# The expert stage in groups of 400 rows instead of 384, with the dense stage left at 384

## What is computed

```python
# x: 3072 tokens x 384, from the attention
logits = x @ w_gate + modality_bias[modality_id]      # 8 experts, 2 modalities
e_idx = np.argmax(logits, axis=1)
for e in range(8):                                    # w1[e]: 384 x 1024, w2[e]: 1024 x 384
    mask = e_idx == e
    h = np.maximum(x[mask] @ w1[e], 0.0)
    out[mask] = gate_w[mask, None] * (h @ w2[e])
# dense stage on all tokens, d_ff = 1536
g = x @ w_gate;  val = x @ w_val
y = (silu(g) * val) @ w_out
```

## Time and profile before

| | us |
|---|---|
| median of three runs | 1021.41 |
| lowest and highest | 1020.64, 1023.75 |
| the profiled execution, its time on the device | 1021.33 |
| its span, first to last instruction | 1019.6 |
| mean granted TensorE clock | 0.975 |

### The profile page before, as it was taken

The page is one execution under the profiler, slowest core; times in us unless marked ns, Lnnn a source line. Parts: engine busy times, 40 slices in busy tenths (PEclk is TensorE's granted clock), DMA queues, the critical chain, the costliest instruction groups (busy, mean ns, idle before and its releaser), DMA issues.

```text
span 1019.6 us, 15885 instructions
## 1 busy us (share of the span) xinstructions
PE 936.1 (92%) x6100; PEld 888.9 (87%) x6100; DVE 579.2 (57%) x993; ACT 382.2 (37%) x536; POOL 175.6 (17%) x198
## 2 busy tenths in 40 slices
PE   2688999999959999999999999999999999999994
PEld 0566878888839999999998999999999999999994
DVE  6978777755566666666555445544444444535432
ACT  7987878756434545444342110111101111011110
POOL 6234234531842211100000001010101000010101
PEclk9799999999959999999999999999999999999998
DMA  9998743420368987765454000000101000000000
GB/s 170 156 156 117 112 88 49 63 56 1 126 215 273 331 280 249 248 201 173 153 187 136 1 24 24 24 24 3 45 1 47 1 24 24 24 24 1 24 1 23
DMA packets 211487, 98.83 MB, mean 97 GB/s; under 512 B 150854, under 2 KB 206406, under 8 KB 211403
## 3 DMA queue, kind: packets, MB, share of 16 engines
q1 hardware_dynamic: 197994, 70.19, 30.3%
q0 software_dynamic: 4368, 14.75, 4.2%
q10 hardware_dynamic: 9040, 12.78, 3.9%
HBM read 77.58 MB, written 20.08 MB: 96 GB/s over the span
## 4 chain that ended last, share of the span: by engine, by line
PE 79%; ACT 5%; DVE 5%; issue 5%; DMA 2%; SPq 2%; POOL 1%; ACTq 0%; DVEq 0%; POOLq 0%
PE psum L1759 27%; PE psum L1771 15%; PE psum L1714 9%; PE psum L1727 9%; PE psum L1568 4%; PE psum L1577 3%; PE psum L1558 2%; PE psum L1613 2%; PE psum L1547 2%; PE psum L1594 2%; PE psum L1616 1%; SPq L587 1%; PE psum L1549 1%; PE psum L1701 1%; ACT group_work L1482 1%
## 5 line engine op out<-in xcount | busy, mean ns | idle before, releaser
L1759 PE MATMUL psum<-xT_parts,w_parts 128*128 128x384 f32 x1728 | 316.3, 335 | 2.3 <-DVE xT_parts L1210 2.3
L1759 PEld LDWEIGHTS psum<-xT_parts,w_parts 128*128 128x128 f32 x1728 | 302.3, 189 | 2.6 <-issue 2.6
L1218 DVE TENSOR_TENSOR group_work<-group_work,psum 128x384 f32<-128x384 f32 x96 | 53.2, 554 | 233.1 <-ACT group_work L1526 233.1
L1526 ACT ACTIVATE group_work<-psum 128x384 f32<-128x384 f32 x96 | 47.2, 492 | 355.3 <-PE psum L1759 355.3
L1771 PE MATMUL psum<-w_parts,act_parts 128*128 128x384 f32 x864 | 166.3, 335 | 5.7 <-DVE act_parts L1226 5.7
L1771 PEld LDWEIGHTS psum<-w_parts,act_parts 128*128 128x128 f32 x864 | 150.7, 188 | 8.4 <-DVE act_parts L1226 8.4
L1714 PE MATMUL psum<-xT_parts,expert_parts 128*128 128x384 f32 x648 | 129.3, 344 | 5.4 <-DVE expert_parts L1167 4.5
L1727 PE MATMUL psum<-act_parts,expert_parts 128*128 128x384 f32 x648 | 123.9, 335 | 0.4 <-DVE act_parts L1172 0.4
L1714 PEld LDWEIGHTS psum<-xT_parts,expert_parts 128*128 128x128 f32 x648 | 113.4, 191 | 8.4 <-DVE expert_parts L1167 6.7
L1727 PEld LDWEIGHTS psum<-act_parts,expert_parts 128*128 128x128 f32 x648 | 112.9, 188 | 1.1 <-DVE act_parts L1172 0.8
L569 POOL DMA_INDIRECT out<-group_work,sorted_id x24 | 23.6, 981 | 462.3 <-ACT group_work L1532 457.4
(11 more groups left out here) (192 smaller groups left out, 1041.6 us busy)
## 6 DMA issues: line engine op xcount, KB each, us to landing
group_work<-in_w SPq DMA_DIRECT2D x160, 192.0 KB, 3.5
group_work<-xs_scratch SPq DMA_DIRECT2D x10, 576.0 KB, 4.7
yT_scratch<-group_work ACTq DMA_DIRECT2D x9, 576.0 KB, 4.4
arena<-in_q SPq DMA_DIRECT2D x24, 192.0 KB, 4.0
arena<-in_k SPq DMA_DIRECT2D x24, 192.0 KB, 4.2
arena<-in_v SPq DMA_DIRECT2D x24, 192.0 KB, 4.4
x_scratch<-x_all SPq DMA_DIRECT2D x24, 192.0 KB, 1.9
xs_scratch<-group_work POOLq DMA_DIRECT2D x8, 576.0 KB, 5.9
```

Of the source, the lines that this page charges most:

```text
L1218: link(nc.vector.tensor_tensor(sig[:, w % 2, :], sig[:, w % 2, :], psum[:, w % 2, 0:GW], ALU.mult))
L1759: last = nc.tensor.matmul(psum[:, b, 0:GW], wt[:, i, k, f * P:(f + 1) * P], x_p[:, j, g % 2, k, :], start=(k == n == 0), stop=(k == KC - 1 ...
```

## The change

- The expert stage has groups of `GE` = `GW` + 16 = 400 rows: matmuls with 400 columns, and ScalarE's and VectorE's operations on `psum`, `x_p` and `act_p` with them. `x_p`, `act_p`, the padding of the scratch tensors and the result buffer `y_sb` (its memory still shared with `osb`) grow; the table is worked out with 400.
- The rows of a group are three tiles of 128 and one of 16 (`xg_last`, sharing memory with `sig`). GpSimd gathers a fourth tile for group 0 and stores it too; the later rounds gather tiles 4 to 6, 7 to 9 and so on, the last one two tiles. `load_rows` has a second DMA of 16 rows. TensorE does a fourth transpose of 16 rows in each `xtr`.
- GpSimd has seven more small operations behind the table, which count the groups that begin in the first 384 columns (times 16), into `tab[3]`.
- The load of the dense stage's first group moves from GpSimd to SyncE, behind all weight loads and behind the nested `If`s of groups 9 and up. It waits for all rows to be sorted and for as many stores as `tab[3]` says.
- The dense stage keeps its 384 columns.

```diff
+    EXTRA = 16
+    GE = GW + EXTRA
...
-                link(nc.gpsimd.tensor_single_scalar(group_pos[:], group_iota_f[:], float(GW), ALU.mult))
+                link(nc.gpsimd.tensor_single_scalar(group_pos[:], group_iota_f[:], float(GE), ALU.mult))
...
-            nc.gpsimd.tensor_copy(tab[0:1, 2, 0:1], sums[:, 1, NE - 1:NE]).then_inc(s_tab, 1)
+            nc.gpsimd.tensor_copy(tab[0:1, 2, 0:1], sums[:, 1, NE - 1:NE])
+            link(nc.gpsimd.memset(begin[:], 0.0))
+            link(nc.gpsimd.tensor_scalar(begin[:, 0:MG], group_at[:], float(GW), 16.0, ALU.is_lt, ALU.mult))
+            half = 8
+            while half >= 1:
+                link(nc.gpsimd.tensor_tensor(begin[:, 0:half], begin[:, 0:half], begin[:, half:2 * half], ALU.add))
+                half //= 2
+            nc.gpsimd.tensor_copy(tab[0:1, 3, 0:1], begin[:, 0:1]).then_inc(s_tab, 1)
...
-            for i in range(TG):
-                pool.indirect_dma_start(xg[:, 0, i], None, x_dram[:, :],
+            for i in range(TG + 1):
+                pool.indirect_dma_start(x_tile(0, i), None, x_dram[:, :],
...
-            pool.wait_ge(s_yst, 16 * NE)
-            pool.dma_start(yT_in, yT_dram[:, 0:GW].rearrange("(k p) n -> p k n", p=P)).then_inc(s_gl0, 16)
+            pool.sem_inc(s_sorted, 1)
...
+                sp.dma_start(xg_last[0:EXTRA, t % 2], xs_dram[ds(first + GW, EXTRA), :]).then_inc(s_xl[t % 2], 16)
...
+            needed = sp.value_load(tab[0:1, 3, 0:1], min_val=16, max_val=16 * NE)
+            sp.wait_ge(s_sorted, 1)
+            sp.wait_ge(s_yst, needed)
+            sp.dma_start(yT_in, yT_dram[:, 0:GW].rearrange("(k p) n -> p k n", p=P)).then_inc(s_gl0, 16)
             stored(NG - 1)
             more_groups(sp, total, NG, NG, stored)
...
-                nc.scalar.activation(act_p[:, 0, w % 2], psum[:, w % 2, 0:GW], ACT.Relu).then_inc(s_hs, 1)
+                nc.scalar.activation(act_p[:, 0, w % 2], psum[:, w % 2, 0:GE], ACT.Relu).then_inc(s_hs, 1)
...
+            def transpose_rows(t, k, i):
+                rows = P if i < TG else EXTRA
+                return nc.tensor.transpose(psum[:, x_bank(t, k), i * P:i * P + rows],
+                                           x_tile(t % 2, i)[0:rows, k * P:(k + 1) * P], ident[0:rows, 0:rows])
...
-                        last = nc.tensor.matmul(psum[:, w % 2, 0:GW], we_p[:, w % SLOTS, i, k * P:(k + 1) * P],
+                        last = nc.tensor.matmul(psum[:, w % 2, 0:GE], we_p[:, w % SLOTS, i, k * P:(k + 1) * P],
                                                 x_p[:, j, t % 2, k, :], start=(k == n == 0),
```

More of the change, by code:

```diff
@@ L81, in build @@
         sorted_id = sb("sorted_id", [P, NT], U32)
-        tab = sb("tab", [1, 4, 32], I32)
+        tab = sb("tab", [1, 4, 16], I32)
         phase = ExitStack()
@@ L302, in build @@
         s_zero = sem("xs_zeroed")
-        s_xf = [sem(f"first_rows{i}_gathered") for i in range(TG)]
+        s_xf = [sem(f"first_rows{i}_gathered") for i in range(TG + 1)]
         s_xs0 = sem("first_rows_stored")
         s_srt = sem("x_rows_sorted")
+        s_sorted = sem("all_rows_sorted")
         s_xs = sem("sorted_rows_stored")
@@ L363, in x_turn, with sorted_tiles, x_tile @@
             return (t + 1, at.index(f)) if f in at and t + 1 < MG else None
+        def sorted_tiles(t):
+            return min(NT, (t + 1) * TG + 1)
+        def x_tile(slot, i):
+            return xg[:, slot, i] if i < TG else xg_last[:, slot]
         w1_v = w1.rearrange("e (k p) f -> p e k f", p=P)
@@ L528, in _ @@
             nc.gpsimd.tensor_copy(tab[0:1, 0, 0:MG], group_e[:]).then_inc(s_te, 1)
-            link(nc.gpsimd.tensor_scalar(small[:, 1, :], sums[:, 0], float(-GW), None, ALU.mult))
+            link(nc.gpsimd.tensor_scalar(small[:, 1, :], sums[:, 0], float(-GE), None, ALU.mult))
             link(nc.gpsimd.tensor_tensor(small[:, 1, :], small[:, 1, :], small[:, 0, :], ALU.add))
@@ L1131, in _ @@
             link(nc.vector.tensor_tensor(small[:, 0, :], cum[0:1, 1:NE + 1], cum[0:1, 0:NE], ALU.subtract))
-            link(nc.vector.tensor_scalar(sums[:, 0], small[:, 0, :], 1.0 / GW, (GW - 1) / 2 / GW, ALU.mult, ALU.add))
+            link(nc.vector.tensor_scalar(sums[:, 0], small[:, 0, :], 1.0 / GE, (GE - 1) / 2 / GE, ALU.mult, ALU.add))
             link(nc.vector.tensor_scalar(sums[:, 0], sums[:, 0], ROUND, -ROUND, ALU.add, ALU.add))
@@ L1207, in split @@
                         dve.wait_ge(s_gv, FFC * (g - 1))
-                high, low = x_p[:, 0, g % 2, k], x_p[:, 1, g % 2, k]
+                high, low = x_p[:, 0, g % 2, k, 0:GW], x_p[:, 1, g % 2, k, 0:GW]
                 link(nc.vector.tensor_copy(high, yT_in[:, k]))
@@ L1223, in _ @@
                         dve.wait_ge(s_o, w - 1)
-                    high, low = act_p[:, 0, w % 2], act_p[:, 1, w % 2]
+                    high, low = act_p[:, 0, w % 2, 0:GW], act_p[:, 1, w % 2, 0:GW]
                     link(nc.vector.tensor_copy(high, sig[:, w % 2]))
@@ L1487, in y_out @@
                     act_e.wait_ge(s_yst, 16 * t)
-                act_e.dma_start(yT_dram[:, ds(first, GW)].rearrange("(k p) n -> p k n", p=P), osb[:, t % 2]
+                act_e.dma_start(yT_dram[:, ds(first, GE)].rearrange("(k p) n -> p k n", p=P), y_sb[:, t % 2]
                                 ).then_inc(s_yst, 16)
@@ L1686, in _ @@
             last.then_inc(s_ids, 1)
+            def transpose_rows(t, k, i):
+                rows = P if i < TG else EXTRA
+                return nc.tensor.transpose(psum[:, x_bank(t, k), i * P:i * P + rows],
+                                           x_tile(t % 2, i)[0:rows, k * P:(k + 1) * P], ident[0:rows, 0:rows])
             def first_rows():
-                for i in range(TG):
+                for i in range(TG + 1):
                     pe.wait_ge(s_xf[i], 16)
                     for k in range(KC):
-                        last = nc.tensor.transpose(psum[:, x_bank(0, k), i * P:(i + 1) * P],
-                                                   xg[:, 0, i, k * P:(k + 1) * P], ident[:])
-                        if i == TG - 1:
+                        last = transpose_rows(0, k, i)
+                        if i == TG:
                             last.then_inc(s_xTp, 1)
             def xtr(t, k):
-                pe.wait_ge(s_xl[t % 2], 16 * ((t + 1) // 2))
+                pe.wait_ge(s_xl[t % 2], 32 * ((t + 1) // 2))
                 pe.wait_ge(s_xT, t * KC + k)
-                for i in range(TG):
-                    last = nc.tensor.transpose(psum[:, x_bank(t, k), i * P:(i + 1) * P], xg[:, t % 2, i, k * P:(k + 1) * P], ident[:])
+                for i in range(TG + 1):
+                    last = transpose_rows(t, k, i)
                 last.then_inc(s_xTp, 1)
@@ L1726, in down @@
                     for n, (i, j) in enumerate(PRODUCTS):
-                        last = nc.tensor.matmul(psum[:, 4 + k, 0:GW], we_p[:, w % SLOTS, i, at:at + P],
+                        last = nc.tensor.matmul(psum[:, 4 + k, 0:GE], we_p[:, w % SLOTS, i, at:at + P],
                                                 act_p[:, j, w % 2], start=(f == n == 0),
```

47 lines of the change are left out of this document (26 added, 21 removed).

## The result

The changed kernel takes 1028.41 us, the median of 20 runs (1024.73 to 1034.04), beside 1021.85 us (1020.64 to 1027.18, 20 runs) for the kernel before: 1.0064 times as long, 95% interval 1.0047 to 1.0080. The forecast was 1014.9 us. The profiled execution took 1027.27 us, with a span of 1025.5. So the change, which takes away a group of 26.7 us, costs 6.6 us.

The account below looks back on a forecast made before the run. TensorE, 92% busy, was taken to bound the kernel; -26.7 + 7.7 + 2.6 + 1.25 + 0.2 - 0.5 + 8.4 + 0.6 = -6.45 us from 1021.33 gave 1014.9 us, range 1009 to 1019.5.

Parts of the forecast that it names:

- What bounds the kernel: TensorE, busy for 92% of the span; dense stage untouched by the change, so the whole question is when it starts.
- Part 1, the ninth group: Expert stage: 400 rows a group need eight groups instead of nine, so the ninth goes; -26.7 us.
- Part 2, sixteen columns: Expert stage: each of 1152 matmuls takes 6.67 ns more for sixteen more columns; +7.7 us (bounds 0 and 8.3).
- 400 columns are a bad width: Rival, at each of the 1152 expert matmuls: paced as if 448 columns, 26.7 ns more, 1038 us; chance 0.06.
- Part 3, the fourth transpose: Expert stage: 24 more transposes on TensorE at 0.11 us each; +2.6 us (bounds 0 and 2.6).
- Part 4, the start: Group 0's fourth gather delays the first `up` by 1.25 us; group 1's rows come later, +0.2 us.
- Part 5, inside each group: Waits of `up` at group ends: cover grows by 0.12 us, the chain by 0.05; -0.5 us over seven.
- Part 6, the handover: Before the dense stage: yT_in's load behind SyncE's weight loads and jump, idle 10.8 us against 2.32; +8.4 us.
- Part 7, the clock: First dense matmuls: lower granted clock after the long handover gap; +0.6 us (bounds -1.0 and +2).

Follow-up runs that it names:

- b_rows400: The kernel before with only the rows of x_p and act_p 400 elements (1600 bytes) apart, still nine groups of 384 columns; 1028.6 us, 1.0068 of before.
- a_align: The changed kernel with rows of x_p 1792 and act_p 2048 bytes apart, single output buffer to make room; 1022.7 us, 0.9989 of before.
- a_16first: The changed kernel with the 16-row transpose issued ahead of the three full ones instead of behind them; 1026.9 us, 1.0054 of before.
- a_k128: The changed kernel with the fourth transpose as a plain 16-column matmul over 128 partitions, tile cleared first by GpSimd; 1027.6 us, 1.0044 of before.
- a_early: The changed kernel with the first yT_in load issued by SyncE in the last group, ahead of its jump; 1022.6 us, 1.0006 of before.
- a_align_early: The changed kernel with aligned rows (1792 and 2048 bytes) and the first yT_in load ahead of SyncE's jump; 1018.0 us, 0.9956 of before.
- a_all: The changed kernel with aligned rows, the fourth transpose over 128 partitions and the first yT_in load ahead of SyncE's jump; 1012.3 us, 0.9885 of before.
- a_align_k128: The changed kernel with aligned rows and the fourth transpose over 128 partitions, first yT_in load still behind SyncE's jump; 1021.6 us, 0.9996 of before.
- a_all2: a_all with GpSimd's clearing of the tile moved ahead of its wait for sorted_id, out from between the gathers; 1010.6 us, 0.9890 of before.

## Why the prediction was wrong, point by point

**What bounds the kernel: the step that failed.** "The dense stage starts there and is untouched by the change, so the whole question is when it starts." Its instructions are untouched, its operands are not: `x_p` and `act_p` are shared by both stages, and their rows grew from 1536 to 1600 bytes. 2592 matmuls at 175.2 instead of 173.4 ns are 4.7 us, the +4.6 of the table, in a stage that the prediction put at nothing. b_rows400 has the loss without the change, and a_align the change without the loss.

**Part 1, the ninth group:** right, 576 matmuls of `up`.

**Part 2, sixteen columns:** the price of the columns was right (7.0 ns in a_align, taken as 6.67). Measured in the changed kernel it is 8.2 ns on average, since the layout adds 1.3 ns here too. Over the 1152 matmuls the 8.2 ns are 1.8 us more than the forecast's 6.67, of which the layout is 1.4: a_align's groups have a period of 28.82 us, 0.18 us shorter than the changed kernel's 29.0, and 8 x 0.18 = 1.4. The rival "400 columns are a bad width" has fallen as it was put: width costs by columns. It was the nearest to the truth in its outcome, slower, and had 0.06. Its place was wrong: most of its loss is in the stage that has 384.

**Part 3, the fourth transpose: the term that was mis-sized.** Taken at 0.11 us, as "fewer columns hardly help", with 2.6 us as the upper bound. It costs (0.49 - 0.33) + (1.82 - 1.64) = 0.34 us, 24 x 0.34 = 8.2 us, of which 5.5 unforeseen. The range was bounded from above by the very row it was taken from. The eight matmuls of the earlier trace rows follow each other with equal shapes; here a 16-row transpose stands between others, and a_16first shows that it costs that much before or behind them. Half of the 0.34 us appears in the row of `up`, which is why the duration of the transposes alone would not have shown it. a_k128 brings it to 0.24. Why the 16-row transpose costs more than the plain matmuls there, no run tells.

**Part 4, the start:** right in itself (+1.1 from the first gather on). The first gather came 1.9 us later in this execution. In the profiled executions of the kernels here, unchanged ones among them, it starts between 293.3 and 295.6 us, so this looks like scatter of the stage before and not like a part of the change. Group 1's rows: 1.52 us of wait instead of 1.08, +0.44 where +0.2 stood. The low clock behind the routing ended 3.5 us after the first `up`, 4.6 us after it in the kernel before, which gave back some 0.5 us; the prediction had no term for that.

**Part 5, inside each group:** right in its sign, taken as -0.5. The seven waits of `up` for `expert_parts` came to 3.5 us where they were 4.5, so it was -1.0.

**Part 6, the handover:** right in size and in its steps. 10.09 us against 10.8. SyncE's last weight load ended at 540.48; the jump took from the branch at 541.1 to 544.15 us, 3.05 us (forecast 3.24); the load took 3.64 (3.9). a_early confirms that the place of the load in SyncE's program is what costs. The bound of 0.8 us above for the jump would not have held in the align kernels, with 4.48 and 4.75 us.

The Trainium skill's two sections stand as they did: the jump's 3.05 us agree with the stall that "Runtime: NRT & Kernel Launch", section Instruction fetch mechanics, describes, and not with the 108 ns of the Control Flow Timing section in "Advanced Engine Details and Errata". That a fetch is what SyncE waits for, no run here shows.

**Part 7, the clock:** right. The first 36 dense matmuls took 8.49 us, 0.58 above; the forecast was 0.6. The low clock covered the first 4.2 us of them, and 3.1 us in the kernel before. The stretch after the handover (length, busy PE, PEld, DVE, ACT, POOL, clock, DMA share, GB/s; against the earlier trace rows):

```profile
543.50:553.80 10.30, 4.24 (x13) 4.27 (x14) 2.58 (x6) 1.28 (x1) 0.00 (x0) 0.50 0.37 114
```

The granted clock fell to its lower level after 4.0 us without a matmul, and 4.2 us after the first dense matmul it was full again.

Together: +4.6 (dense stage) + 5.5 (transposes) + 1.8 (pace of the expert stage) + 0.2 (group 1's rows) - 0.5 (waits inside the groups) - 0.5 (low clock at the start) + 1.9 (scatter ahead) - 0.7 (handover) - 0.1 (from the first gather on) = 12.2 of the 12.4 us. The two large misses stand where the forecast had nothing (the dense stage) and where it had taken its upper bound (the transposes).

**What stays open.** *How* the layout slows matmuls. An equal shift of all four tensors by 64 bytes is free, rows of 1792 and 2048 bytes are as good as 1536 with the tensors where a_align has them, and rows of 1600 are not. A shift of two tensors by 64 bytes, with rows of 1536, slows one line of four. No rule for it is shown. *What stops TensorE after five dense matmuls* (3.17 and 2.64 us, with no wait in the record): it is there in both kernels that load early without k128, and in neither of the two with it. These two have 27 matmuls and 27 weight loads more in TensorE's program ahead of that place (6001 matmuls against 5974), so the same instruction stands elsewhere in it; whether that is what counts, no run tells. Nor is it known why SyncE's jump takes 4.5 to 4.8 us in the two align kernels that load late, which is 1.4 to 1.7 of the 2 us by which their idle time before the dense stage is longer than in the changed one.

## What to carry to other kernels

A buffer that two stages share carries a change of shape from one to the other: look where every operand of the longest stage lies before and after, and when a width changes, measure the pace of the untouched stage too: rows padded to 1792 and 2048 bytes brought it back here. Price a small odd-shaped instruction from its neighbours in place, with what the instruction behind it loses, and never let the row from which a term is taken be its upper bound. Here the change was worth 1.1% once the layout, the odd transpose and the place of the first load were mended, and cost 0.6% without.

## What the runs showed of the hardware that was not expected

- The pace of a matmul of fp32r operands depends on where they lie: 173.3 to 173.5 ns for 384 columns in the layout before, 175.2 to 175.8 in others, with the same instructions. For 400 columns it is 180.3 to 180.4 (a_align), and 181.3 to 182.1 in the changed kernel.
- A transpose of 16 rows between full ones and float32r matmuls costs 0.34 us, three times a full one (0.11). As a plain 16-column matmul over 128 partitions, which runs as two instructions, it costs 0.21 to 0.24 us.
- A taken jump over unused groups stops SyncE for 3.05 to 3.24 us in the changed kernel, a_16first, a_k128 and the kernel before, and for 4.48 and 4.75 us in the two align kernels that load late.
- How long TensorE had been idle did not by itself tell whether the granted clock fell: it fell behind 3.26 us (a_k128) and 2.46 us (a_align_early) at group 1's rows and behind 2.32 us before the dense stage (the kernel before), and stayed full behind 2.33 and 2.34 us at group 1's rows (a_all, a_align_k128) and 3.00 us before the dense stage (a_all2).
